# The load queue in odd steps: two weight blocks ahead of the wait for the remainder of q

## What is computed

```
scores = q k^T / sqrt(D), causal;  a = softmax(scores);  local = a v        # B=4, H=8, S=576, D=64
q_p = elu(q) + 1;  mem = (q_p M_prev) / (q_p . z_prev + 1e-6)
x = sigmoid(beta) * mem + (1 - sigmoid(beta)) * local                        # -> (2304, 512)
x = (sigmoid(x w_gate) * (x w_val)) w_out                                    # d_ff 1536
h = x w_in;  out = (h * clip(h + 3, 0, 6) / 6) w_out2                        # d_ff 2048
```

## Time and profile before

| | us |
|---|---|
| median of 3 runs | 1107.15 (1106.24 to 1109.83) |
| profiled execution, its own time | 1103.73 |
| its span | 1101.9 |
| TensorE matmuls busy | 1058.2 (96%) |
| TensorE weight loads busy | 994.1 (90%) |
| VectorE busy | 711.7 (65%) |
| ScalarE busy | 636.9 (58%) |
| GpSimd busy | 532.6 (48%) |
| mean granted TensorE clock | 0.991 |

### The profile page before, as it was taken

The page is one execution under the profiler, slowest core; times in us unless marked ns, Lnnn a source line. Parts: engine busy times, 40 slices in busy tenths (PEclk is TensorE's granted clock), DMA queues, the critical chain, the costliest instruction groups (busy, mean ns, idle before and its releaser), DMA issues.

```text
span 1101.9 us, 20594 instructions
## 1 busy us (share of the span) xinstructions
PE 1058.2 (96%) x6740; PEld 994.1 (90%) x6740; DVE 711.7 (65%) x1543; ACT 636.9 (58%) x1436; POOL 532.6 (48%) x560
## 2 busy tenths in 40 slices
PE   5999999998999999999999999999999999999998
PEld 4778999998999999999999999988898889888987
DVE  5997766766867767668565444475678556665553
ACT  5787676676766766767655443455555433453333
POOL 5996566556755665666554664237882011000000
PEclk9999999999999999999999999999999999999999
DMA  8553332432343333424322435334545544454421
GB/s 187 136 133 96 90 108 73 122 107 75 95 125 96 94 99 95 117 67 112 86 60 75 125 105 169 129 117 153 189 143 165 180 116 123 113 174 118 122 58 58
DMA packets 126348, 126.90 MB, mean 115 GB/s; under 512 B 12080, under 2 KB 92464, under 8 KB 126000
## 3 DMA queue, kind: packets, MB, share of 16 engines
q1 hardware_dynamic: 125968, 122.07, 39.7%
q10 hardware_dynamic: 288, 3.67, 0.9%
HBM read 106.30 MB, written 19.40 MB: 114 GB/s over the span
## 4 chain that ended last, share of the span: by engine, by line
PE 84%; DVE 5%; DMA 4%; issue 3%; ACT 2%; SPq 1%; ACTq 0%; DVEq 0%
PE ps L808 80%; DMA stage<-w_val 4%; PE ps L849 3%; DVE q_s L1470 1%; SPq L437 1%; PE ps L862 1%; DVE prob L1562 1%; DVE pt_lo L1509 1%; ACT pt_hi L1151 0%; DMA qk_st<-qk_t 0%; DVE phit L1509 0%; DVE phi L1543 0%; DVE Cb L1759 0%; ACT WG L1179 0%; DVE Y L1730 0%
## 5 line engine op out<-in xcount | busy, mean ns | idle before, releaser
L808 PE MATMUL ps<-x_hi,WG 128*128 128x288 f32 x1536 | 328.4, 300 | 17.1 <-DVE pt_lo L1509 17.0
L808 PEld LDWEIGHTS ps<-x_hi,WG 128*128 128x128 f32 x1536 | 255.2, 191 | 20.0 <-issue 11.4
L808 PE MATMUL ps<-x_lo,WG 128*128 128x288 f32 x768 | 228.7, 298 | 0.0
L808 PE MATMUL ps<-XC,WC 128*128 128x384 f32 x1008 | 202.5, 336 | 2.1 <-DVE Cb L1759 1.7
L808 PEld LDWEIGHTS ps<-XC,WC 128*128 128x128 f32 x1008 | 180.3, 188 | 17.7 <-issue 3.2
L665 POOL TENSOR_TENSOR WG<-stage,WG 128x512 fp32r<-128x512 f32 x96 | 122.9, 1294 | 134.4 <-ACT WG L1179 134.3
L808 PE MATMUL ps<-h_hi,WO 128*128 128x288 f32 x768 | 166.9, 300 | 4.8 <-DVE Y L1732 4.7
L808 PE MATMUL ps<-wo,G_hi 128*128 128x512 f32 x540 | 168.0, 392 | 0.0
L808 PEld LDWEIGHTS ps<-x_lo,WG 128*128 128x128 f32 x768 | 146.8, 191 | 0.5
L1759 DVE TENSOR_TENSOR Cb<-ps,Cb 128x384 f32<-128x384 f32 x168 | 89.2, 554 | 83.3 <-PE ps L808 81.4
L693 POOL TENSOR_SCALAR prob<-prob,rscale 128x128 f32<-128x128 f32 (+4 forms) x160 | 103.6, 665 | 74.5 <-DVE rscale L1521 74.5
(11 more groups left out here) (137 smaller groups left out, 1959.8 us busy)
## 6 DMA issues: line engine op xcount, KB each, us to landing
WC<-w_in_parts SPq DMA_DIRECT2D x112, 256.0 KB, 2.7
stage<-w_out SPq DMA_DIRECT2D x64, 256.0 KB, 3.1
qk_st<-qk_t SPq DMA_DIRECT2D x54, 288.0 KB, 4.2
stage<-w_gate SPq DMA_DIRECT2D x48, 256.0 KB, 3.4
stage<-w_val SPq DMA_DIRECT2D x48, 256.0 KB, 3.2
w_in_parts<-WC SPq DMA_DIRECT2D x42, 256.0 KB, 2.0
qn_st<-q_n SPq DMA_DIRECT2D x16, 256.0 KB, 3.4
w_in_parts<-WC ACTq DMA_DIRECT2D x2, 1792.0 KB, 7.4
```

What stands on the lines that cost most here:

```text
L808: return pe.matmul(o, l, r, start=start, stop=stop, skip_group_check=True)
```

## The change

The condition for loading the next q and k gets a name and the load a function. In an even step it is called where it stood. In an odd step it is called inside the loop over the weight blocks, ahead of the third (x == 2), so after blocks 5 and 6 and before blocks 7 and 8.

```diff
@@ -479,10 +479,15 @@
                 if scoring and p == 1 and not is_last(n, p):
                     ready(phizd, n + 1)
                     load_phi(n + 1)
-                if scoring and not is_last(n, p) and not is_last(n + p, 1 - p):
+                more_qk = scoring and not is_last(n, p) and not is_last(n + p, 1 - p)
+
+                def next_qk():
                     ready(q_ready, u + 2)
                     ready(k_ready, u + 2)
                     load_qk(u + 2)
+
+                if more_qk and p == 0:
+                    next_qk()
                 prep = prepared(r) if r is not None and not (scoring or old) and p == 0 else None
                 if prep == 0:
                     sp.wait_ge(x_done, n_heads)
@@ -491,6 +496,8 @@
                     load_raw_in(1)
                 if r is not None:
                     for x, (ahead, k) in enumerate([x for slot in CUT[p] for x in slot]):
+                        if x == 2 and more_qk and p == 1:
+                            next_qk()
                         more, k = divmod(k + NST, BLK)
                         more += ahead
                         if not more:
```

## The result

| | before | after |
|---|---|---|
| median, us | 1106.84 (1106.24 to 1109.83) | 1076.73 (1074.07 to 1077.33) |
| profiled execution, its own time | 1103.73 | 1076.30 |
| its span | 1101.9 | 1074.5 |
| mean granted clock | 0.991 | 0.998 |

The median before is 1106.84 here and not 1107.15, since one more execution (1106.53) has come to the three. The ratio is 0.9718 (95% interval 0.9694 to 0.9742): 30.1 us faster. (Lines behind the edit moved by 7 in the changed kernel: L1509 is now L1516, L1179 L1186, L1732 L1739, L808 L815, L849 L856.)

The account below looks back on a forecast made before the run. TensorE's matmuls were taken to bound the kernel, with ten waits hanging on late w_val loads. Waits 18.3 + clock 6.2 = 24.5 us off the profiled 1103.73 gives 1079.2, plus the 3.4 offset 1082.6 us; range 1077 to 1094.

Parts of the forecast that it names:

- Place and mechanism: Odd steps of pairs 5 to 14: block 5 loads earlier, ScalarE's 3.96 us wait and TensorE's ten waits go.
- 2.8 taken: Landing time in us assumed for block 5's load with nothing in front, as in pair 15's odd step.
- 40.3 was said: Time in us forecast for a changed pair without a clock drop.
- not 6: Likely cover in us before ScalarE wants the moved q and k load; 1.8 in the worst case.
- The 1.4 of the prediction: Cover in us between VectorE's L1509 done at 350.4 and TensorE wanting it at 351.8, pair 10.
- the slow landing: Block 5 landing after 4.4 us, at 348.7 in pair 10, said to use 0.5 us of the 1.4 cover.
- The correction for each wait, +0.13: At TensorE's ten waits for L1509: time returned beyond the row's length, 1.3 us over ten, bound 0 to 0.2 each.
- The clock, four drops of 1.55: Behind the ten waits for L1509: four lower-clock stretches of 1.55 us each go, returning 6.2 us.
- both would stay: Pairs 8 and 12: the two clock drops behind TensorE's waits for L1732 (Y) were to remain.
- The same difference from it: Whole kernel: 3.4 us, median above profiled execution, carried over from 1079.2 to give 1082.6.
- The range: Forecast range for the whole kernel's time: 1077 to 1094 us.
- The rule of the Trainium skill that was weighed: Attention stage: waits too short to lower the clock, so it returns nothing; rival 1, 1088.9 us, chance 0.16.

Follow-up runs that it names:

- The delayed kernels: Changed kernel with ScalarE repeating its copy of block 5 two, four or eight times in each of the ten steps: 1077.0, 1086.01 and 1127.77 us.
- two repeats: Changed kernel with ScalarE repeating its copy of block 5 twice in each of the ten steps: 1077.0 us.
- The third profile of before: The kernel before, unchanged, profiled a third time: 1107.19 us.
- the second and fourth profile: The kernel before, unchanged, profiled a second and a fourth time: 1104.99 and 1105.29 us.
- eight repeats: Changed kernel with ScalarE repeating its copy of block 5 eight times in each of the ten steps: 1127.77 us, ratio 1.0182.
- with no wait left: Changed kernel with GpSimd's remainders of the middle x tiles held back until VectorE's remainder of q is done, in pairs 8 and 12: 1069.42 us.

## Why the prediction was off in size

Point by point, by its own steps.

- *Place and mechanism*: right. ScalarE's wait of 3.96 is gone, the load goes first and lands in 2.9 us (2.8 taken), all ten waits of TensorE are gone, the plain pair takes 40.17 (40.3 was said), q and k leave at the same point and nobody waits for them; their cover is some 4 us, not 6. The delayed kernels show that it was ScalarE's delay that was at work, and that TensorE feels it beyond a cover of some 2 us (held up by 2.61 us it waits 0.3 to 0.75). The 1.4 of the prediction are the part of it behind VectorE: the remainder of tile 2 ends at 336.10, 1.5 before TensorE's 337.59. Another 0.8 lie between ScalarE's copy (ends 334.75) and VectorE's start (335.55). So the slow landing would not have used 0.5 of the 1.4, as was said: by the prediction's own rows VectorE is with the Y addition until 349.81 in any case.
- *The correction for each wait, +0.13*: mis-sized. A plain pair without drops went from 42.26 to 40.17 us, 2.09 for a wait whose row says 1.84: 0.25 each. I had allowed 0 to 0.2. Over ten waits 1.2 us more than the 1.3 taken.
- *The clock, four drops of 1.55*: the size was right (pair 6: 43.64 to 40.17 is 3.47, less the wait of 1.69 and 0.25 leaves 1.53), the number was not. Five went, since one of the two behind the waits for Y did not come either: 1.5 us. Which of these come differs by execution; the four other profiles with the new queue and both waits for Y, up to two repeats, have 1, 0, 0 and 1. That this helped the profiled execution is luck; that both would stay was not to be relied on.
- With both the sum for the profiled execution is 27.2, and 27.4 was measured.
- *"The same difference from it"*: the step that failed, and the largest term of the miss. I moved the 3.4 us by which the median lay above the profiled execution over to the changed kernel as if they were a constant. The changed kernel's profiled execution is 0.4 us from its median: 3.0 us. Without them, and with the 2.7 us of the two terms above, the forecast would have been 1076.9. Either error alone would have left the time inside the range. The third profile of before, 3.5 us above the first, shows what such an offset can be made of: two more drops behind the ten waits and some 0.6 us of longer waits. For executions without a profile the granted clock points the same way: the profiles with six drops have 0.991, the third 0.989, and 17 of the 27 executions of before beside the experiments have 0.989 or less. It is not all of it: the second and fourth profile have as many drops as the first and lie 1.3 and 1.6 us above it, of which 0.4 and 0.5 are a later start of pair 5, on which the change does nothing. How the 3.4 us divide between these parts stays open.
- *The range*: the prediction puts the clock at up to 15.5 us, 9.3 more than the 6.2 in its sum, and says that this stays in the range. It does not: 1082.6 less 9.3 is 1073.3, and the range ended at 1077.0, with two or three drops more and nothing for the resuming or the offset.
- The rule of the Trainium skill that was weighed, "TensorE: Matmul & The Clock Gate", section "HAM oscillation — how this bites in real kernels" (only longer idle stretches lower the clock): the runs decide against it here. 38 of 67 waits of 1.5 to 2.7 us were followed by a drop; the table is in the last section.

## What to carry to other kernels

Read for each load on a critical wait what stands ahead of it in its issuing queue, and whether its own buffer has been free before that; the q and k load had some 4 us of slack and the weight block none. Credit a removed wait of TensorE with its row, the resuming (0.25 us here), and the clock drops behind it, unless a later wait takes the drop up, as in pair 12. And where an offset between profile and median is to be carried over, ask what it is made of: if it hangs on the wait that goes, it goes too.

## What the runs showed of the hardware

**The clock falls behind short waits, at some lengths in one execution and not in the next.** Over thirteen profiles (the eleven runs told of here, before and after), each wait of TensorE between pairs 5 and 15, with whether the granted clock fell to 0.50 near its end:

| wait of TensorE | waits | followed by a drop |
|---|---|---|
| 0.15 to 0.8 us | 23 | 0 |
| 1.5 to 2.7 us | 67 | 38 |
| 2.9 to 3.2 us | 9 | 9 |

In the middle class the drop begins between 0.7 us before TensorE resumes (the wait of 2.59 us that ends at 461.30 with eight repeats) and 1.6 us after it (1.5 at 353.76); the example is the wait for Y that ends at 416.66 in the changed kernel (columns as in the earlier trace rows):

```profile
416.00:417.00 1.00, 0.34 (x1) 0.34 (x2) 1.00 (x4) 1.00 (x3) 0.00 (x0) 0.78 0.66 97
417.00:418.00 1.00, 1.00 (x5) 1.00 (x5) 0.64 (x2) 1.00 (x3) 0.08 (x1) 0.50 0.78 263
418.00:419.00 1.00, 1.00 (x6) 0.98 (x6) 0.00 (x0) 1.00 (x3) 1.00 (x1) 0.50 0.93 221
```

It lasts 3.4 us and costs 1.5; four lasted 6.8, behind waits of 2.59 to 3.21 us. Between pairs 5 and 15 no drop was seen without such a wait. Executions of one kernel differ in which waits are followed by one, and that makes up part of their spread: 1102 to 1110 us before, 1074 to 1077 after, 1069.0 to 1070.2 with no wait left.

**VectorE and GpSimd wait for each other in SBUF.** VectorE's remainder of q took 1.86 us beside GpSimd's remainder and 0.76 once that was held back; its remainder of x 2.06 and 0.75. The Trainium skill, page "SBUF — State Buffer", section "Who interferes with whom", has the two engines share a pair of ports under an exclusive lock, and has a VectorE instruction with two SBUF inputs contend with a GpSimd instruction that reads SBUF. All four here are of that kind, and the trace agrees: both VectorE rows together take 3.92 us instead of 1.51, and GpSimd's two took 3.33 us instead of 2.83. From the first start to the last end the four take 3.95 us (247.80 to 251.75), little less than the 4.34 of one after the other. VectorE's L1516, whose other operand is in PSUM, kept its length beside GpSimd's low parts (0.55 us in pair 10, the mean of its 24).
